# Channel attention with a feed-forward layer: keys issued from one queue, and a first chunk of one row

## The chip, the cores and the metric

The kernel runs on one core of a Trainium2 chip. The metric is the device time of one execution in microseconds (us), the median of several executions. The kernel before takes 1074.12 us (three runs, 1074.07 to 1074.76).

The engines are called PE (matrix multiplication), ACT (activations and copies), DVE and POOL (elementwise work), and SP, which here only issues DMA transfers. PEld is the weight load that goes ahead of each matmul. "ACTq" and "SPq" rows are the issuing of transfers by these engines.

## What is computed

```
q, k, v: (2, 6016, 256) float32;  w_in: (256, 2048);  w_out: (2048, 256)
qn = q / (norm of q over axis 1 + 1e-6);  kn likewise
s  = kn^T @ qn / tau                 # (2, 256, 256), one matrix per batch
a  = softmax of s over the last axis
x  = v @ a                           # (2, 6016, 256), seen as 12032 tokens
h  = x @ w_in;  out = (h * sigmoid(h)) @ w_out
```

## The kernel before, in words

The program has two parts. The **scoring part** (to about 84 us of the span) reads all queries and keys once, adds up the 256 x 256 scores and the sums of squares for the norms. The **token part** (the rest) folds the softmax of each batch into w_in and sends the tokens through both layers in 12 steps of 8 pairs of matrix products. In the token part the order of each engine's work is fixed, and PE's matmuls follow each other.

In the scoring part a batch has 47 "rows": a row is 128 partitions x 256 channels of the queries and the same of the keys, 128 KB each. Rows go in chunks. `HEADS` (L55) gives the rows of a batch's first chunks and every other chunk has 3 rows, so batch 0 is cut into 2, 3, 3, ... (16 chunks) and batch 1 likewise; chunks are numbered 0 to 31 and called c0, c1, ... here. A chunk's queries are one transfer and its keys another, into one of 9 slots of a ring (the slots carry the names qk, wp_raw and home in the trace: chunk 5 and 6 go to wp_raw, 7 and 8 to home, then 9 to 13 to qk, and so on). From c9 on a load waits until the chunk nine before has been scored and squared.

All transfers of the scoring part are issued by SP (L287 queries, L289 keys), but for the keys of c0, c1 and c2, which ACT issues before its first work (L770 and L771, `KEYS_BY_ACT = 3`). Behind some chunks SP also issues parts of w_in, tau and the first tokens (`W_IN_BEHIND`, `TAU_BEHIND`, `TOKENS_BEHIND`, all chunk numbers).

For each chunk in order, ACT squares queries and keys into PSUM (L630), and DVE adds the squares to a running sum (L846); the two take turns over two PSUM areas. PE scores a chunk in one of two ways. A plain chunk takes two float32 matmuls of 256 columns per row (L434, each shown as two records). A **split** chunk (the keys of `LATE`: 5, 8, 11, 14, 17, 20, 21, 23, 27) is rounded by ACT (L676), its remainder is taken by POOL (L354), and PE scores it from the parts (L449 to L456). `LATE[g]` says after how many further chunks PE comes back to it: c5 is scored behind c7, c14 behind c15.

Before any data is there, PE runs `WARM = 7` float32 matmuls of a matrix of ones by itself (L585; 14 records), whose result nothing reads.

Of the kernel before, what the change touches and what calls it, by code (L numbers as in the profile page):

```python
# [11 lines left out]
P = 128  # L12
BANK = 512
# [3 lines left out]
TOK = 512  # L17
NARROW = 448

KEYS_BY_ACT = 3  # L20
WARM = 7


LATE = {5: 2, 8: 2, 11: 2, 14: 1, 17: 3, 20: 2, 21: 5, 23: 5, 27: 4}
SPLIT = tuple(LATE)

W_IN_BEHIND = (17, 24, 26, 28)
TAU_BEHIND = 11
TOKENS_BEHIND = 22
SETS = 2  # L30


# [8 lines left out]
def channel_attention_ffn(nc, q, k, v_t, tau, w_in, w_out, out_t):  # L41
# [6 lines left out]
    B, N, C = q.shape  # L48
    F = w_in.shape[1]
    CK = C // P  # L50
    FK = F // P
    PAIRS = FK // 2
    R = N // P

    HEADS = ((2,), (2,))  # L55
    CHUNKS = []
    for b in range(B):
        row = 0
        for rows in HEADS[b] + (ROWS,) * ((R - sum(HEADS[b])) // ROWS):
            CHUNKS.append((b, row, rows))  # L60
            row += rows
        assert row == R
    ENDS = [sum(b <= last for b, _, _ in CHUNKS) for last in range(B)]
    SECOND = ENDS[0]

    ORDER = sorted(range(len(CHUNKS)), key=lambda g: (g + LATE[g], 1) if g in SPLIT else (g, 0))
    PLACE = [ORDER.index(g) for g in range(len(CHUNKS))]
    assert all(CHUNKS[g][2] == ROWS and CHUNKS[g][0] == CHUNKS[g + LATE[g]][0] for g in SPLIT)
    assert [g for g in ORDER if g in SPLIT] == list(SPLIT)
    WIDE = N // (2 * TOK)  # L70
    STEPS = WIDE + 1
    ALL = B * STEPS
    FOLDS = CK * (F // BANK)
    PARTS = 4
    assert B == 2 and N % P == 0 and N == 2 * (TOK * WIDE + NARROW) and NARROW % 2 == 0
    assert C == 2 * P and PAIRS == 8 and FOLDS == 8 and F == PARTS * BANK and STEPS == 6 and ENDS == [16, 32] and TOK <= BANK

    with ExitStack() as ctx:
        def sb(name, shape, dt=F32, stack=ctx):
            return stack.enter_context(nc.sbuf_tensor(name, shape, dt))  # L80

        def sem(name):
            return ctx.enter_context(nc.semaphore(name))
# [40 lines left out]
        with ExitStack() as early:  # L124
            qk = [sb(f"qk{s}", [P, 2, ROWS, C], stack=early) for s in range(RING - 4)]
# [60 lines left out]
        slot_loaded = [sem(f"slot_loaded{s}") for s in range(RING)]  # L186
# [63 lines left out]
        def rows_of(x, g):  # L250

            b, row, rows = CHUNKS[g]
            return x[b, row * P:(row + rows) * P, :].rearrange("(p r) c -> p r c", r=rows)
# [6 lines left out]
        def w_in_part(w, n):  # L260
            return w[:, :, n * BANK:(n + 1) * BANK]

        def tokens_of(step):

            return 2 * TOK * (step % STEPS), TOK if step % STEPS < WIDE else NARROW
# [10 lines left out]
        @block.sync  # L276
        def _(sp):
            def load_chunk(g):
                rows = CHUNKS[g][2]
                s = g % RING  # L280
                if g >= RING:
                    if g - RING in SPLIT:
                        sp.wait_ge(rows_split, SPLIT.index(g - RING) + 1)
                    else:
                        sp.wait_ge(chunk_scored, PLACE[g - RING] + 1)
                    sp.wait_ge(chunk_squared, 2 * (g - RING + 1))
                sp.dma_start(qk[s][:, 0, 0:rows, :], rows_of(q, g)).then_inc(slot_loaded[s], 16)  # L287
                if g >= KEYS_BY_ACT:
                    sp.dma_start(qk[s][:, 1, 0:rows, :], rows_of(k, g)).then_inc(slot_loaded[s], 16)  # L289

            def load_v(step):

                first, n = tokens_of(step)
                for i, (c, t) in enumerate(((0, 1), (0, 0), (1, 0), (1, 1))):
                    sp.dma_start(v_raw[:, i, 0:n], v_t[step // STEPS, c * P:(c + 1) * P,
                                                       first + t * n:first + (t + 1) * n]).then_inc(v_loaded, 16)

            sp.sem_inc(out_stored, 32)
            w_out_parts = w_out.rearrange("(n f p) c -> n p f c", p=P, n=PARTS)
            w_in_parts = w_in.rearrange("(c p) (n f) -> n p c f", p=P, f=BANK)  # L300
            for g in range(len(CHUNKS)):
                load_chunk(g)
                if g in W_IN_BEHIND:
                    n = W_IN_BEHIND.index(g)
                    sp.dma_start(w_in_part(w_in_raw, n), w_in_parts[n]).then_inc(w_in_loaded[n], 16)
                if g == TAU_BEHIND:
                    sp.dma_start(tau_col[:], bass.AP(tau.tensor, 0, [[0, P], [1, 1]])).then_inc(tau_loaded, 16)
                if g == TOKENS_BEHIND:
                    load_v(0)
            for n in range(PARTS):  # L310
                sp.dma_start(wo_raw[:, n * FK // PARTS:(n + 1) * FK // PARTS, :], w_out_parts[n]).then_inc(
                    wo_loaded[n], 16)
            sp.wait_ge(v_split, 3)
            load_v(1)

            def out_half(step, t):
                first, n = tokens_of(step)
                first += step // STEPS * N + t * n
                return out_t.rearrange("(c p) n -> p c n", p=P)[:, :, first:first + n]

            for step in range(ALL - 1):

                n = tokens_of(step)[1]
                for late, t in enumerate((1, 0)):
                    sp.wait_ge(out_copied, 2 * step + late + 3)
                    sp.dma_start(out_half(step, t), out_sb[:, t, :, 0:n]).then_inc(out_stored, 16)
                if step < ALL - 2:

                    sp.wait_ge(out_stored, 32 * step + 64)
                    load_v(step + 2)  # L330
            for late, t in enumerate((1, 0)):
                last = out_half(ALL - 1, t)
                sp.wait_ge(last_copied_dve, late + 1)
                sp.dma_start(last[:, 0, :], out_sb[:, t, 0, 0:NARROW]).then_inc(out_stored, 16)
                if late == 0:
                    sp.wait_ge(last_copied_act, 1)
                    sp.dma_start(last[:, 1, :], out_sb[:, t, 1, 0:NARROW]).then_inc(out_stored, 16)

            sp.wait_ge(out_stored, 32 * ALL + 64)
# [87 lines left out]
        def _(pe):  # L427
# [155 lines left out]
            pe.wait_ge(consts_made, 1)  # L583
            for n in range(WARM):
                nc.tensor.matmul(ps_turn[:, 0:P], ones[:], ones[:], start=True, stop=True)  # L585
# [37 lines left out]
        def _(act):  # L623
# [143 lines left out]

            act.sem_inc(silu_11, 1)
            act.sem_inc(out_copied, 2)
            for g in range(KEYS_BY_ACT):  # L770
                act.dma_start(qk[g][:, 1, 0:CHUNKS[g][2], :], rows_of(k, g)).then_inc(slot_loaded[g], 16)  # L771
            for g in range(len(CHUNKS)):
                square_chunk(g)
                if g in SPLIT:
# [286 lines left out]
```

## Time and profile before

| what | value |
|---|---|
| median of three runs | 1074.12 us |
| the profiled execution, its own time | 1073.79 us |
| its span in the profile | 1072.0 us |
| PE busy | 1067.4 us of the span |
| DVE, ACT, POOL busy | 729.7, 633.8, 61.9 us |
| moved by DMA | 54.08 MB, 361, 398 and 358 GB/s in the first three of 40 slices |

The span begins with the first instruction that the profiler records and ends with the last; the execution's own time has 1.79 us more around it. POOL's work lies in the scoring part alone. A row of a timeline gives the start, the time from the first start to the last end of the merged instructions, the engine, the line, the operation with its tiles, and in brackets how long the engine had been idle before and what ended the wait. Ends of matmuls are modelled, so neighbouring PE rows overlap a little.

### The profile page before, as it was taken

What the parts mean: (1) busy time and instruction counts of PE and PEld (TensorE: products, weight loads), DVE (VectorE), ACT (ScalarE), POOL (GpSimd) and SP (SyncE); (2) the same over time, 40 slices, a digit from 0 to 9 for tenths busy, and PEclk for the clock granted to TensorE, in tenths of its full rate; (3) what the DMA queues carried; (4) which work ended last, traced back from release to release, by engine and by line L of the source; (5) the groups of instructions that cost most, each with busy time, mean ns of one, the idle gap of its engine ahead of it and who ended that gap; (6) DMA issues with size and microseconds to landing.
All of it is one profiled execution on the core that took longest, in us unless ns stands there. A gap on an engine that the chain in (4) does not pass through costs nothing.

```text
span 1072.0 us, 13049 instructions
## 1 busy us (share of the span) xinstructions
PE 1067.4 (100%) x4850; PEld 902.8 (84%) x4850; DVE 729.7 (68%) x939; ACT 633.8 (59%) x787; POOL 61.9 (6%) x33
## 2 busy tenths in 40 slices
PE   9999999999999999999999999999999999999998
PEld 8988888888888888888999888888888888888998
DVE  6889787567566566566788776667567566566665
ACT  7998665555555555555666655555555555555554
POOL 3692000000000000000000000000000000000000
PEclk9999999999999999999999999999999999999999
DMA  9991000200200200200200200200200200200100
GB/s 361 398 358 40 1 1 1 79 1 1 79 1 0 78 0 0 73 0 0 80 1 0 74 1 1 79 1 1 79 1 1 78 0 0 73 0 0 40 1 35
DMA packets 26077, 54.08 MB, mean 50 GB/s; under 512 B 2480, under 2 KB 6576, under 8 KB 26032
## 3 DMA queue, kind: packets, MB, share of 16 engines
q1 hardware_dynamic: 25456, 52.21, 13.4%
q10 hardware_dynamic: 576, 1.28, 0.3%
q8 instruction: 27, 0.44, 0.2%
q14 instruction: 18, 0.15, 0.0%
HBM read 41.16 MB, written 12.32 MB: 50 GB/s over the span
## 4 chain that ended last, share of the span: by engine, by line
PE 99%; DMA 1%; ACT 0%; ACTq 0%; issue 0%
PE ps_o L529 16%; PE ps_o L530 16%; PE ps_o L531 16%; PE ps_h L495 14%; PE ps_h L496 14%; PE ps_h L494 14%; PE ps_o L434 5%; PE ps_o L449 1%; PE ps_o L456 1%; DMA qk<-k_dram 1%; PE ps_h L486 0%; PE ps_h L488 0%; PE ps_h L487 0%; PE ps_o L488 0%; PE ps_o L487 0%; PE ps_o L486 0%
## 5 line engine op out<-in xcount | busy, mean ns | idle before, releaser
L496 PE MATMUL ps_h<-b_hi,a_lo_rest 128*128 128x512 f32 (+1 forms) x504 | 194.1, 385 | 0.0
L495 PE MATMUL ps_h<-b_lo,a_hi_rest 128*128 128x512 f32 (+1 forms) x504 | 194.1, 385 | 0.0
L494 PE MATMUL ps_h<-b_hi,a_hi_rest 128*128 128x512 f32 (+1 forms) x504 | 194.0, 385 | 0.0
L978 DVE TENSOR_TENSOR h_b<-ps_h,u 128x512 f32<-128x512 f32 x96 | 66.4, 692 | 161.5 <-PE ps_h L496 161.4
L956 DVE TENSOR_TENSOR u<-ps_h,u 128x512 f32<-128x512 f32 x96 | 66.4, 692 | 142.9 <-PE ps_h L496 91.7
L750 ACT ACTIVATE h_a<-ps_h 128x512 f32<-128x512 f32 x96 | 57.4, 598 | 161.9 <-PE ps_h L496 161.8
L530 PE MATMUL ps_o<-g_lo_a,wo_hi 128*128 128x512 f32 (+1 forms) x384 | 147.9, 385 | 0.0
L529 PE MATMUL ps_o<-g_hi_b,wo_hi 128*128 128x512 f32 (+1 forms) x384 | 147.9, 385 | 0.0
L531 PE MATMUL ps_o<-g_hi_b,wo_lo 128*128 128x512 f32 (+1 forms) x384 | 147.9, 385 | 0.0
L529 PE MATMUL ps_o<-g_hi_a,wo_hi 128*128 128x512 f32 (+1 forms) x384 | 147.9, 385 | 0.0
L530 PE MATMUL ps_o<-g_lo_b,wo_hi 128*128 128x512 f32 (+1 forms) x384 | 147.8, 385 | 0.0
L531 PE MATMUL ps_o<-g_hi_a,wo_lo 128*128 128x512 f32 (+1 forms) x384 | 147.8, 385 | 0.0
L760 ACT ACTIVATE h_b<-h_b 128x1024 f32<-128x1024 f32 x96 | 102.0, 1063 | 42.6 <-DVE h_b L980 42.6
L728 ACT ACTIVATE u<-ps_h 128x512 f32<-128x512 f32 x96 | 57.3, 597 | 115.8 <-PE ps_h L496 115.7
L982 DVE TENSOR_TENSOR g_lo_a<-h_a,g_hi_a 128x1024 fp32r<-128x1024 f32 x96 | 116.8, 1217 | 1.6 <-ACT g_hi_a L754 1.6
L949 DVE TENSOR_TENSOR g_lo_b<-h_b,g_hi_b 128x1024 fp32r<-128x1024 f32 x95 | 115.4, 1215 | 0.0
L747 ACT ACTIVATE h_a<-h_a 128x512 f32<-128x512 f32 x96 | 60.8, 633 | 91.5 <-DVE h_a L963 91.3
L494 PEld LDWEIGHTS ps_h<-b_hi,a_hi_rest 128*128 128x128 f32 x504 | 94.6, 188 | 17.7
L496 PEld LDWEIGHTS ps_h<-b_hi,a_lo_rest 128*128 128x128 f32 x504 | 94.6, 188 | 17.6
L495 PEld LDWEIGHTS ps_h<-b_lo,a_hi_rest 128*128 128x128 f32 x504 | 94.6, 188 | 17.6
L754 ACT ACTIVATE g_hi_a<-h_a 128x1024 fp32r<-128x1024 f32 x96 | 101.9, 1062 | 4.6
L705 ACT ACTIVATE g_hi_b<-h_b 128x1024 fp32r<-128x1024 f32 x95 | 100.1, 1054 | 0.0
(140 smaller groups left out, 1601.3 us busy)
## 6 DMA issues: line engine op xcount, KB each, us to landing
v_raw<-v_t_dram SPq DMA_DIRECT2D x40, 256.0 KB, 3.6
out_t_dram<-v_raw SPq DMA_DIRECT2D x20, 512.0 KB, 3.2
qk<-q_dram SPq DMA_DIRECT2D x19, 384.0 KB, 10.6
qk<-k_dram SPq DMA_DIRECT2D x17, 384.0 KB, 12.2
wp_raw<-q_dram SPq DMA_DIRECT2D x6, 384.0 KB, 10.3
wp_raw<-k_dram SPq DMA_DIRECT2D x6, 384.0 KB, 10.9
w_in_raw<-w_in_dram SPq DMA_DIRECT2D x4, 512.0 KB, 11.9
wo_raw<-w_out_dram SPq DMA_DIRECT2D x4, 512.0 KB, 12.3
```

What stands on the lines that cost most here:

```text
L494: nc.tensor.matmul(ps_h[:, bank, 0:n], w_hi, x_hi, start=start, stop=False, skip_group_check=True)
L495: nc.tensor.matmul(ps_h[:, bank, 0:n], w_hi, x_lo, start=False, stop=False, skip_group_check=True)
L496: return nc.tensor.matmul(ps_h[:, bank, 0:n], w_lo, x_hi, start=False, stop=stop, skip_group_check=True)
L529: nc.tensor.matmul(out, wo_hi[:, block_, d], g_hi[:, i, 0:tok], start=start, stop=False)
L530: nc.tensor.matmul(out, wo_hi[:, block_, d], g_lo[:, i, 0:tok], start=False, stop=False)
L531: return nc.tensor.matmul(out, wo_lo[:, block_, d], g_hi[:, i, 0:tok], start=False, stop=stop)
L705: nc.scalar.activation(g_hi_b[:], h_b[:], ACT.Copy).then_inc(hi_b, 1)
L754: nc.scalar.activation(g_hi_a[:], h_a[:], ACT.Copy).then_inc(hi_a, 1)
L760: nc.scalar.activation(h_b[:], h_b[:], ACT.Silu).then_inc(silu_b, 1)
L949: nc.vector.tensor_tensor(g_lo_b[:], h_b[:], g_hi_b[:].bitcast(F32), ALU.subtract).then_inc(lo_b, 1)
L956: nc.vector.tensor_tensor(u[:], ps_h[:, BANK_P6, :], u[:], ALU.add).then_inc(u_made, 1)
L982: nc.vector.tensor_tensor(g_lo_a[:], h_a[:], g_hi_a[:].bitcast(F32), ALU.subtract).then_inc(lo_a, 1)
```

## The change

Three things, with the tables of chunk numbers moved along. All keys are issued by SP, each behind its chunk's queries. Batch 0 opens with chunks of 1, 2 and 2 rows in place of 2 and 3, so that it has 17 chunks, and every later chunk keeps its rows and gets a number one higher (c2 before is n3 now; chunks of the changed kernel are called n0, n1, ... here). PE runs five matmuls of ones ahead, not seven.

```diff
-KEYS_BY_ACT = 3
-WARM = 7
-LATE = {5: 2, 8: 2, 11: 2, 14: 1, 17: 3, 20: 2, 21: 5, 23: 5, 27: 4}
+WARM = 5
+LATE = {6: 2, 9: 2, 12: 2, 15: 1, 18: 3, 21: 2, 22: 5, 24: 5, 28: 4}
...
-W_IN_BEHIND = (17, 24, 26, 28)
-TAU_BEHIND = 11
-TOKENS_BEHIND = 22
+W_IN_BEHIND = (18, 25, 27, 29)
+TAU_BEHIND = 12
+TOKENS_BEHIND = 23
...
-    HEADS = ((2,), (2,))
+    HEADS = ((1, 2, 2), (2,))
...
                 sp.dma_start(qk[s][:, 0, 0:rows, :], rows_of(q, g)).then_inc(slot_loaded[s], 16)
-                if g >= KEYS_BY_ACT:
-                    sp.dma_start(qk[s][:, 1, 0:rows, :], rows_of(k, g)).then_inc(slot_loaded[s], 16)
+                sp.dma_start(qk[s][:, 1, 0:rows, :], rows_of(k, g)).then_inc(slot_loaded[s], 16)
...
-            for g in range(KEYS_BY_ACT):
-                act.dma_start(qk[g][:, 1, 0:CHUNKS[g][2], :], rows_of(k, g)).then_inc(slot_loaded[g], 16)
```

On SP, at the start of the program, the order before is this (128x512 is two rows, 128x768 three):

```order
L287 DMA qk<-q_dram 128x512
L287 DMA qk<-q_dram 128x768 x3
L289 DMA qk<-k_dram 128x768
L287 DMA qk<-q_dram 128x768
L289 DMA qk<-k_dram 128x768
L287 DMA wp_raw<-q_dram 128x768
```

And the same place on SP in the changed program:

```order
L286 DMA qk<-q_dram 128x256
L287 DMA qk<-k_dram 128x256
L286 DMA qk<-q_dram 128x512
L287 DMA qk<-k_dram 128x512
L286 DMA qk<-q_dram 128x512
L287 DMA qk<-k_dram 128x512
L286 DMA qk<-q_dram 128x768
L287 DMA qk<-k_dram 128x768
```

SP now issues queries and keys in turn from the first chunk on, and has issued six transfers with five rows where it had issued four with eleven rows of queries.

On ACT, at the start of the program, before:

```order
L771 DMA qk<-k_dram 128x512
L771 DMA qk<-k_dram 128x768 x2
L630 ACT_TABLE_LOAD
L630 ACTIVATE ps_h<-qk 128x512 x2
L630 ACTIVATE ps_h<-qk 128x768 x8
```

And the same place on ACT in the changed program:

```order
L628 ACT_TABLE_LOAD
L628 ACTIVATE ps_h<-qk 128x256 x2
L628 ACTIVATE ps_h<-qk 128x512 x4
L628 ACTIVATE ps_h<-qk 128x768 x4
```

The three issues ahead of the table load are gone, and the squares come in three small chunks and then in chunks of three rows.

## Rows read from the trace of the kernel before

**Rows 1.** The page: busy time of each engine over the span.
```profile
PE 1067.4 (100%) x4850; PEld 902.8 (84%) x4850; DVE 729.7 (68%) x939; ACT 633.8 (59%) x787; POOL 61.9 (6%) x33
```

**Rows 2.** Waits of PE: whom it waited for, us in total, times, longest.
```profile
PE ps_o L585 <- POOL ones L343: 1.1, 1, 1.1
PE ps_o L434 <- DMA qk<-k_dram: 0.4, 2, 0.2
```

**Rows 3.** Timeline of PE, the opening.
```profile
1.07 3.33 PE L585 MATMUL ps_o<-ones 128*128 128x128 f32 x14 [1.07 <-POOL ones L343]
4.57 1.99 PE L434 MATMUL ps_o<-qk 128*128 128x256 f32 x8 [0.17 <-DMA qk<-k_dram]
6.78 10.63 PE L434 MATMUL ps_o<-qk 128*128 128x256 f32 x48 [0.21 <-DMA qk<-k_dram]
17.24 2.75 PE L434 MATMUL ps_o<-wp_raw 128*128 128x256 f32 x12
```

**Rows 4.** Timeline of SP's and ACT's issuing, the opening.
```profile
0.81 1.81 SPq L287 DMA_DIRECT2D qk<-q_dram  x4
0.89 1.35 ACTq L771 DMA_DIRECT2D qk<-k_dram  x3
2.66 0.74 SPq L289 DMA_DIRECT2D qk<-k_dram  x1
4.89 0.43 SPq L289 DMA_DIRECT2D wp_raw<-k_dram  x1
5.84 0.43 SPq L289 DMA_DIRECT2D wp_raw<-k_dram  x1
```

**Rows 5.** DMA issues by short windows: size, us to landing; c0, c1, c2 from ACT.
```profile
qk<-k_dram ACTq DMA_DIRECT2D x1, 256.0 KB, 3.6
...
qk<-k_dram ACTq DMA_DIRECT2D x1, 384.0 KB, 5.4
...
qk<-k_dram ACTq DMA_DIRECT2D x1, 384.0 KB, 7.0
```

**Rows 6.** The same for SP's keys of c3, c5 and c6.
```profile
qk<-k_dram SPq DMA_DIRECT2D x1, 384.0 KB, 7.8
...
wp_raw<-k_dram SPq DMA_DIRECT2D x1, 384.0 KB, 9.4
...
wp_raw<-k_dram SPq DMA_DIRECT2D x1, 384.0 KB, 10.5
```

**Rows 7.** Tile v_raw at 87 to 95 us: four 256 KB loads on idle queues.
```profile
L295 SPq DMA_DIRECT2D v_raw<-v_t_dram x4: 340/432/432, 88.6 to 89.9; - x4
...
DMA to landing us min/median/max: 2.6/3.3/4.5
```

**Rows 8.** Timeline of ACT: table load, squares of c0, c2 and c5.
```profile
2.27 1.28 ACT L630 ACT_TABLE_LOAD   x1 [2.27 <-issue]
4.55 1.12 ACT L630 ACTIVATE ps_h<-qk 128x512 f32<-128x512 f32 x2 [1.00 <-DMA qk<-k_dram]
...
8.78 1.55 ACT L630 ACTIVATE ps_h<-qk 128x768 f32<-128x768 f32 x2 [0.48 <-DMA qk<-k_dram]
...
14.48 0.81 ACT L630 ACTIVATE ps_h<-wp_raw 128x768 f32<-128x768 f32 x1 [0.28 <-DVE square_sum L846]
```

**Rows 9.** Timeline of POOL: the remainders of c14, and of c20 with c21.
```profile
37.70 3.48 POOL L354 TENSOR_TENSOR qk_parts<-wp_raw,qk_parts 128x1536 fp32r<-128x1536 f32 x1 [3.22 <-ACT qk_parts L676]
...
52.24 6.95 POOL L354 TENSOR_TENSOR qk_parts<-qk,qk_parts 128x1536 fp32r<-128x1536 f32 x2 [1.60 <-ACT qk_parts L676]
```

**Rows 10.** Timeline of PE's weight loads: the first of c14, the first of c20.
```profile
41.62 0.19 PEld L452 LDWEIGHTS ps_o<-qk_parts 128*128 128x128 f32 x1
...
56.27 0.19 PEld L449 LDWEIGHTS ps_o<-qk_parts 128*128 128x128 f32 x1
```

**Rows 11.** Weight loads by tile: count, ns min/median/max, first and last start.
```profile
L585 PEld LDWEIGHTS ps_o<-ones x14: 289/333/338, 1.0 to 3.8; 128*128 128x128 f32 x14
...
L434 PEld LDWEIGHTS ps_o<-qk x33: 186/190/190, 4.6 to 11.8; 128*128 128x128 f32 x33
```

**Rows 12.** Mean granted clock by windows (after the PE, PEld, DVE, ACT, POOL columns).
```profile
3.00:4.00 1.00, 1.00 (x7) 1.00 (x6) 0.00 (x0) 0.55 (x1) 1.00 (x1) 1.00 0.98 381
4.00:5.00 1.00, 0.83 (x4) 0.51 (x4) 0.00 (x0) 0.45 (x1) 0.25 (x1) 1.00 1.04 413
```

More of the change, by code:

```diff
@@ L75, in channel_attention_ffn @@
     assert B == 2 and N % P == 0 and N == 2 * (TOK * WIDE + NARROW) and NARROW % 2 == 0
-    assert C == 2 * P and PAIRS == 8 and FOLDS == 8 and F == PARTS * BANK and STEPS == 6 and ENDS == [16, 32] and TOK <= BANK
+    assert C == 2 * P and PAIRS == 8 and FOLDS == 8 and F == PARTS * BANK and STEPS == 6 and ENDS == [17, 33] and TOK <= BANK
     with ExitStack() as ctx:
```

## The prediction

> **What bounds the kernel now.** The page comes first: PE is busy for 1067.4 of 1072.0 us [rows 1], so only 4.6 us of the span are PE's idle time, and no change of order can win more than that without removing matmuls. The list of PE's waits comes next: it holds three waits only, one of 1.1 us for the ones to be written and 0.4 us, in two pieces, for keys [rows 2]. The timeline says where they lie. PE multiplies ones until 4.40, scores c0 from 4.57 and c1 from 6.78, and from there never waits again: c1 to c4, four chunks with 12 rows, take 6.78 to 17.24, which is 0.872 us a row and 2.615 a chunk [rows 3]. So the end of the kernel is the time at which PE's unbroken stream starts, plus its work. This change leaves the work as it is (the same 94 rows, the same parts) and can only move the start. The rest of the argument is whether what feeds PE (transfers, then ACT's rounding, then POOL's remainders) can follow if PE comes earlier.
>
> **When the data lands now.** A landing is the issue time plus the time to landing. ACT issues its three keys from 0.89, 0.45 us apart [rows 4], and they land at 4.49 (c0), 6.74 (c1) and 8.79 (c2) [rows 5]; PE at 4.57 and 6.78 and ACT's squares at 8.78 start just there [rows 3, 8]. Keys from SP: c3 at 2.66 + 7.8 = 10.46, c5 at 4.89 + 9.4 = 14.29, c6 at 5.84 + 10.5 = 16.34 [rows 4, 6]. From c3 to c6 nine rows arrive in 5.88 us: 0.653 us a row. That is a stream that is full all the time, and the change moves the same bytes through it. Carried back from c3 (11 rows landed), the line gives 8.50 for 8 rows, 6.54 for 5, 5.24 for 3 and 3.93 for one. What really landed was 0.3 and 0.2 us behind this line for c2 and c1, since queries of later chunks went beside their keys.
>
> **The change, part by part.**
>
> *Keys from SP, in order.* The keys of n0, n1, n2 and n3 are SP's 2nd, 4th, 6th and 8th issues. Four issues took 1.81 us [rows 4], 0.45 each, so n1's keys go out at 0.81 + 3 x 0.45 = 2.17 where those of c1 went at 1.34. For their landing no row exists; the bounds are 2.17 + 2.6 = 4.77, by the quickest of four loads of 256 KB on idle queues [rows 7], and 6.74, where c1's keys landed now. I take 5.24, by the line of the full stream, since it also meets c0 (4.58 for two rows against 4.49 measured). In the same way n0 is complete at 3.93, n2 at 6.54 and n3 at 8.50. Against the move speaks only the issuing. The Trainium skill (DMA: Bandwidth & Descriptors, "Issuing engines are not separate DMA queues") says that issuing on several engines saves just the sequencer's time and that all transfers share the same 16 DMA engines; by that rule nothing is lost, and the sum stays. SP's own queue gets five more issues ahead of n7's, about 2.3 us; they are covered by the backlog, as c6's keys waited 10.5 us [rows 6] and leave about 7.9 now to land at 16.34. Without that backlog all starts behind would be up to 2.3 us later.
>
> *Chunks of 1, 2 and 2 rows.* PE starts n0 at 3.93. Its row costs 0.87 at the full clock and 1.74 at half; if the clock rises at about 4.3 it ends at 5.0, before n1 is there. n1 runs from 5.24 to 6.98, n2 (landed 6.54) to 8.73, n3 (landed 8.50) starts at 8.73. Before, the same rows (c2) start at 6.78 + 2.615 = 9.40. **Gain at the front: 0.67 us.** It is n1's landing that sets this, not n0's. The added chunk costs PE nothing and ACT about 0.7 us of squares (1.12 for two rows, 1.55 for three [rows 8]), DVE about as much, between 3.9 and 5.2, where both wait for n1. The table load begins near 0.9 in place of 2.27 and ends before n0 lands either way: nothing. n9's new wait is on n0, done long before. The shifted tables name the same data as before: nothing.
>
> *Five pairs of ones.* Each record took 0.214 us, so ten end near 3.55 in place of 4.40, before n0 lands. Nothing is won but that they are out of n0's way; with seven pairs n1 would still wait for 5.24. What it may cost is in the rivals.
>
> *Does the rest follow?* c6 starts at 17.24 and landed at 16.34: 0.90 us of room, enough for 0.67. The split chunks are tighter. POOL's remainder of c14 ends at 37.70 + 3.48 = 41.18 and PE's first weight load of it is at 41.62: 0.44. For c20 it is 52.24 + 3.48 = 55.72 and 56.27: 0.55 [rows 9, 10]. POOL waits for ACT there, and ACT squares c5 at 14.48, when its keys had landed at 14.29: ACT can come 0.19 earlier and no more, as the transfers do not come sooner. So PE can gain 0.44 + 0.19 = 0.63 at c14. With a little slower start of a single queue taken off, I put **the net at 0.55 us**: what is late next is POOL's remainder of c14, on which PE waits for the first time. Behind 84 us everything hangs on PE's own stream and shifts with it.
>
> **Sum.** Against the profiled execution: 1073.79 - 0.55 = 1073.24. The median of the runs stands 0.33 above that execution, so **1073.6 us**. A measurement of this kernel can tell about 0.2%, 2.15 us, from no change; the forecast is inside that.
>
> **The rivals.**
>
> *The clock rises late (slower).* The granted clock reads 1.00 from the start [rows 12], but the weight loads tell otherwise: 333 ns for the ones, 190 from c0's first on, with one of 289 last among the ones [rows 11]. So PE ran at 1.2 GHz until about 4 us and at 2.4 from 4.57, after more than 3 us of unbroken matmuls. Now it would be busy from 1.07 to 3.55 and have holes at 3.55 to 3.93 and before n1. With the rise at time T, n0 takes 3.93 to 5.67, and n1 and n2 (3.49 us of work) end at 6.33 + T/2; against 9.40 that is a loss from T = 6.15 on. A rise 3.5 us late, at 8.0, ends them at 10.33: 0.9 lost, 1075.0. Only from T = 10.5 would the loss pass 2.15. For it: fewer ones and the holes. Against it: the holes are short, and real matmuls go on. The Trainium skill (TensorE: Matmul & The Clock Gate, "Part 1") says that the default state is throttled and activity releases it, which would make this the danger of the change. Chance 0.10, and 0.03 of them beyond 10.5.
>
> *The single queue starts slower.* SP's first two issues carry 128 KB each in 0.45 us, 0.29 MB/us, under the 0.40 at which the stream then runs. If the whole line is 0.4 us later, n1 starts at 5.64, the front gains 0.27, and c14 leaves 0.44 - 0.21 = 0.23: 1073.9 to 1074.1. At the upper bound of n1's landing (6.74, the line 1.5 late) 0.8 is lost. The Trainium skill's rule (DMA: Bandwidth & Descriptors, "Rules for kernel authors") to use 1 MiB or more per transfer for bandwidth speaks for this rival; the trace has nothing under 256 KB here. Chance 0.17.
>
> *More than the forecast.* Small transfers on otherwise idle queues land nearer to 4.8 for n1, and POOL and ACT give more room than their modelled ends show. Then the front gains up to 0.90, where c6's landing stops it: 1073.1. Chance 0.13.
>
> *The change does not do what it says.* n0 may land no sooner than c0 did, 4.49, if a landing is mostly latency. Then n0 ends at 5.36, n1 starts 0.1 later, and the net is 0.5 still: no time of its own.
>
> **How the numbers follow.** Forecast 0.57, more 0.13, slow queue 0.17, late clock 0.10, and 0.03 for what I do not see. All but the far end of the late clock lie within 2.15 us, and the largest gain the rows allow is under 1 us: faster 0.02, same 0.94, slower 0.04. The range holds forecast, slow queue, more, and most of the late clock with the runs' own spread of 0.3: 1072.8 to 1074.9.
>
> **What would show it.** PE's row of n0 near 3.9, of n1 near 5.2, of n3's rows near 8.7; the landings of SP's keys on the line 3.93, 5.24, 6.54, 8.50. A first wait of PE for POOL at c14 (n15 now), of a tenth or two, and ACT's squares of n6 at 14.3. Weight loads of 190 ns from the second half of n0 on. The prediction is wrong if n1's keys land after 6, if weight loads of 333 ns go on past n1, or if PE waits more than half a microsecond for POOL or ACT.

## The result, and the profile after

The changed kernel takes **1075.97 us** (median of 22 runs, 1075.11 to 1076.51) where the kernel before takes 1074.13 (22 runs, 1073.57 to 1074.76): 1.84 us slower, a ratio of 1.0017 with the interval 1.001 to 1.0023. The forecast was 1073.6, with a range to 1074.9. The time lies outside it and went the other way. The loss is inside the 0.2% up to which the forecast spoke of "same", but the interval leaves out a ratio of 1, so it is a loss and not noise. The profiled execution took 1076.3 us with a span of 1074.5, 2.5 us more span than before.

PE's list of waits in the changed kernel (us in total, times, longest), where [rows 2] stood before:

```profile
PE ps_o L432 <- DMA qk<-k_dram: 1.2, 2, 0.9
PE ps_o L583 <- POOL ones L341: 1.1, 1, 1.1
PE ps_o L472 <- ACT scores L645: 0.6, 1, 0.6
PE ps_o L461 <- DVE square_sum L848: 0.3, 1, 0.3
```

Two waits are new, both far behind the chunks that were changed: for ACT's exponentials and for DVE's sum of squares, in the softmax of batch 1. The opening of PE, in answer to [rows 3]:

```profile
1.07 2.47 PE L583 MATMUL ps_o<-ones 128*128 128x128 f32 x10 [1.07 <-POOL ones L341]
3.36 1.91 PE L432 MATMUL ps_o<-qk 128*128 128x256 f32 x4
5.66 3.72 PE L432 MATMUL ps_o<-qk 128*128 128x256 f32 x16 [0.39 <-DMA qk<-k_dram]
10.23 5.45 PE L432 MATMUL ps_o<-qk 128*128 128x256 f32 x24 [0.85 <-DMA qk<-k_dram]
15.51 2.75 PE L432 MATMUL ps_o<-wp_raw 128*128 128x256 f32 x12
```

n0 starts at 3.36, even sooner than forecast, and n1 at 5.66. But n3, the first chunk of three rows, starts at 10.23: 1.5 us later than forecast and about 0.8 later than the same rows (c2) before, which start at 9.40 by the forecast's working and at 9.47 by their first record. The cause is to be read from the landings. These are the keys of n0 to n4 from SP's queue, each asked for in its own short window (KB, us to landing), as [rows 5, 6]:

```profile
qk<-k_dram SPq DMA_DIRECT2D x1, 128.0 KB, 2.1
...
qk<-k_dram SPq DMA_DIRECT2D x1, 256.0 KB, 3.4
...
qk<-k_dram SPq DMA_DIRECT2D x1, 256.0 KB, 4.1
...
qk<-k_dram SPq DMA_DIRECT2D x1, 384.0 KB, 6.1
...
qk<-k_dram SPq DMA_DIRECT2D x1, 384.0 KB, 7.1
```

Issued at 1.25, 2.18, 3.13, 4.08 and 5.03, they land at 3.35, 5.58, 7.23, 10.18 and 12.13. The forecast line had 3.93, 5.24, 6.54, 8.50 and 10.46. So one row came earlier, and from three rows on each landing is later, up to 1.7 us for 8 and 11 rows. The windows of the opening (last column GB/s, the one before it the share of the DMA engines that is busy) show a thin stream where it had 381, 413, 406, 415 and 403 GB/s from 3 to 8 us before:

```profile
3.00:4.00 1.00, 1.00 (x5) 0.81 (x5) 0.17 (x1) 0.67 (x2) 1.00 (x1) 1.00 0.72 178
4.00:5.00 1.00, 1.00 (x4) 0.62 (x2) 0.59 (x2) 0.03 (x1) 0.25 (x1) 1.00 1.05 399
5.00:6.00 1.00, 0.61 (x4) 0.32 (x3) 0.00 (x0) 0.37 (x1) 0.00 (x0) 1.00 0.94 292
6.00:7.00 1.00, 1.00 (x6) 0.90 (x5) 0.73 (x2) 0.75 (x2) 0.00 (x0) 1.00 1.08 373
7.00:8.00 1.00, 1.00 (x7) 0.87 (x6) 0.70 (x2) 0.78 (x2) 0.00 (x0) 1.00 0.94 341
```

Only a part of this is idle time of the DMA engines: their busy shares add up to 4.73 of these 5 us in place of 5.10 before, 7% less, while the bytes are 22% fewer (1.58 MB in place of 2.02). The rest is packets that took longer. From 9 us on the stream moves as fast as before, but what it missed stays missed. Added up, the windows to 8 us have moved 1.87 MB in place of 2.27. These 0.40 MB are 1.0 us of the full stream, so the thin stream makes about 1.0 of the 1.67 us by which the keys of 11 rows are late. For the rest, 3.56 MB had moved by that landing where it was 3.28 MB before: bytes of later chunks went ahead of it. ACT squares n6 at 16.12 where c5 had 14.48, and POOL takes every remainder 1.56 us later. At n15, the c14 of [rows 9, 10], the room of 0.44 us is gone (timelines of POOL and of the weight loads):

```profile
39.26 3.48 POOL L352 TENSOR_TENSOR qk_parts<-wp_raw,qk_parts 128x1536 fp32r<-128x1536 f32 x1 [3.25 <-ACT qk_parts L674]
...
42.80 0.19 PEld L450 LDWEIGHTS ps_o<-qk_parts 128*128 128x128 f32 x1 [0.27 <-POOL qk_parts L352]
```

PE waits 0.27 us there and is 1.06 us late behind it (n17 at 45.05 where c16 had 43.99). At the last split chunk it is 1.10 late (82.22 against 81.12). The other 1.4 us of the 2.5 arise between 82 and 97 us. This is DVE, then POOL, before (the last squares are added until 81.2, L851 and L852 add up the three rows, L878 begins the softmax sums of batch 0; POOL's L396, L366 and L401 take remainders that PE needs later):

```profile
81.20 2.05 DVE L851 TENSOR_TENSOR square_sum<-square_sum 128x512 f32<-128x512 f32 x1
83.28 0.69 DVE L852 TENSOR_TENSOR square_sum<-square_sum 128x512 f32<-128x512 f32 x1
83.89 2.37 DVE L878 TENSOR_SCALAR row_sum<-row_sum 128x2 f32<-128x2 f32 x1
```

```profile
80.29 2.41 POOL L396 TENSOR_TENSOR b_lo<-t_raw,b_hi 128x1024 fp32r<-128x1024 f32 x1
83.63 2.60 POOL L366 TENSOR_TENSOR w_in_lo<-w_in_raw,w_in_hi 128x1024 fp32r<-128x1024 f32 x1 [0.94 <-ACT w_in_hi L686]
86.19 2.37 POOL L401 TENSOR_TENSOR b_lo<-v_raw,b_hi 128x1024 fp32r<-128x1024 f32 x1
```

And the same in the changed kernel (L847 and L848 are the additions, L874 the softmax sums):

```profile
82.26 2.54 DVE L847 TENSOR_TENSOR square_sum<-square_sum 128x512 f32<-128x512 f32 x1
84.84 2.81 DVE L848 TENSOR_TENSOR square_sum<-square_sum 128x512 f32<-128x512 f32 x1
87.57 2.33 DVE L874 TENSOR_SCALAR row_sum<-row_sum 128x2 f32<-128x2 f32 x1
```

```profile
81.87 2.38 POOL L394 TENSOR_TENSOR b_lo<-t_raw,b_hi 128x1024 fp32r<-128x1024 f32 x1
84.69 2.40 POOL L364 TENSOR_TENSOR w_in_lo<-w_in_raw,w_in_hi 128x1024 fp32r<-128x1024 f32 x1 [0.44 <-ACT w_in_hi L684]
87.06 2.81 POOL L399 TENSOR_TENSOR b_lo<-v_raw,b_hi 128x1024 fp32r<-128x1024 f32 x1
```

Compare the durations. One addition over 128x512 takes 0.69 us by itself. When one of POOL's instructions is under way as it starts, it ends 0.55 us after POOL's does (83.25 and 82.70, 87.65 and 87.09), and so takes 2.05 to 2.81 us here. A sum over 128x2 takes 2.3 us in the same company, ends 0.03 us after POOL's instruction, and takes 0.16 alone, as an experiment below shows. POOL's instruction is the longer one when it comes second: 2.60 us for L366 at 83.63 and 2.81 for L399 at 87.06, where the others of this size take about 2.4. So the two engines take turns. Before, the second addition started at 83.28, in the gap that POOL left between 82.70 and 83.63; it missed POOL's next instruction by 0.35 us. In the changed kernel POOL leaves only 0.44 us (84.25 to 84.69), the first addition ends behind the gap, and the second waits for a whole instruction of POOL, the third for one more. DVE's scaling of the scores begins at 90.72 in place of 87.71, the exponentials at 95.19 in place of 92.18, and PE, which had folds to do meanwhile, runs out of them at 95.8. The Trainium skill (SBUF — State Buffer, "Who interferes with whom") states this as a rule: DVE and GpSimd (POOL here) share one pair of SBUF ports as an exclusive lock, a DVE instruction with two SBUF inputs contends for it with a GpSimd instruction that reads SBUF, and so does DVE in a two-port mode, where whoever issues first blocks the other for the whole instruction. The trace agrees, with 0.69 against 2.81 us.

### The profile page after: what moved, and what is told of

Its sections match the earlier page's. It is cut to its first block, busy times and chain, and to the rows that moved or that the text cites. A ratio compares the mean times of both kernels' runs of the same rounds, so it can differ in the third digit from the quotient of the medians.

```text
span 1074.5 us, 13051 instructions
## 1 busy us (share of the span) xinstructions
PE 1068.1 (99%) x4846; PEld 902.2 (84%) x4846; DVE 732.1 (68%) x941; ACT 633.7 (59%) x789; POOL 62.1 (6%) x33
## 4 chain that ended last, share of the span: by engine, by line
PE 91%; ACT 4%; DVE 2%; issue 1%; DMA 1%; SPq 1%; ACTq 0%
PE ps_o L527 16%; PE ps_o L528 16%; PE ps_o L529 16%; PE ps_h L493 14%; PE ps_h L494 14%; PE ps_h L492 14%; ACT ps_h L628 3%; DVE square_sum L842 1%; DMA wp_raw<-k_dram 1%; ACT qk_parts L674 0%; PE ps_o L486 0%; PE ps_o L484 0%; PE ps_o L485 0%; SPq L286 0%; DVE square_sum L848 0%
## 6 DMA issues: line engine op xcount, KB each, us to landing
wp_raw<-q_dram SPq DMA_DIRECT2D x7, 384.0 KB, 10.4
w_in_raw<-w_in_dram SPq DMA_DIRECT2D x4, 512.0 KB, 11.5
```

## The experiments

Medians are of 11 runs each; the kernel before had 1074.03, 1074.11 and 1073.96 in the three sets, of 33 runs each. The brackets give the ratio to it and the ratio's interval, which is about 0.001 wide on either side, 1 us, so that differences are read together with the traces. Three theories stood at first. *One queue* and *small chunks* say that the transfers come late, by the one or the other part of the change; *clock* says that fewer ones cost it.

**Keys from SP alone.** Chunks and ones as before.

```diff
-KEYS_BY_ACT = 3
+KEYS_BY_ACT = 0
```

> The kernel before, with all keys issued by SP behind their queries, chunks of 2 and 3 rows and seven pairs of ones as before. Theory 'one queue' (the transfers of the first microseconds run dry because one engine issues them all): 1.0 to 2.0 us slower than before, c3's keys land after 11.2 us where they landed at 10.5. Theory 'small chunks' (an issue takes 0.45 us whatever it carries, so 128 and 256 KB transfers leave holes): within 0.4 us of before. Theory 'clock': within 0.4 us of before, no weight load of 333 ns after 5 us.

Measured: 1074.84 (1.0005, 0.9996 to 1.0015). PE's opening, and three windows of the transfers:

```profile
4.44 2.55 PE L434 MATMUL ps_o<-qk 128*128 128x256 f32 x8
8.48 10.63 PE L434 MATMUL ps_o<-qk 128*128 128x256 f32 x48 [1.49 <-DMA qk<-k_dram]
```

```profile
4.00:5.00 1.00, 1.00 0.94 266
5.00:6.00 1.00, 1.00 1.09 277
6.00:7.00 1.00, 1.00 0.78 277
```

(The windows have only the granted clock, the share and the GB/s.) c1 starts at 8.48 where it started at 6.78, and the stream is thin there with transfers of 256 and 384 KB too. So this edit alone makes the first landings late: c3's keys land at 12.36 us, past the 11.2 that this theory named. The median is 0.81 us above before, less than the profile's 1.7 us (the profiled execution took 1075.53) and less than the theory wanted, and the interval still holds a ratio of 1. The edit changes two things at once, the queue of three transfers and the order in which queries and keys enter (each chunk's keys now go ahead of the next chunk's queries); no run separates them. Each issue carries 256 KB or more in 0.47 us here, above the rate of the stream, so the pace of issuing is not what makes the stream thin.

**Small chunks alone.** The heads of the change, keys of the first three chunks by ACT, seven pairs of ones.

```diff
-    HEADS = ((2,), (2,))
+    HEADS = ((1, 2, 2), (2,))
```

> The kernel before, with batch 0 opening with chunks of 1, 2 and 2 rows, keys of the first three chunks still issued by ACT, seven pairs of ones. Theory 'one queue': no slower than before, perhaps 0.5 us faster. Theory 'small chunks': 1.0 to 2.0 us slower, the keys of the fourth chunk (8 rows in) land after 9.5 us. Theory 'clock': within 0.4 us of before.

Measured: 1074.81 (1.0009, 1.0 to 1.0019). PE's row of n2:

```profile
8.52 7.17 PE L434 MATMUL ps_o<-qk 128*128 128x256 f32 x32 [0.24 <-DMA qk<-k_dram]
```

n2 starts at 8.52 and n3 two rows later, against 9.40 for the same rows before; the keys of 11 rows land at 11.5 in place of 10.46. The keys of 8 rows land at 9.55, at the edge of what the theory of small chunks named. So this part makes the landings late too; the median is 0.78 us above before, less than the theory wanted, with an interval that begins at 1. Neither theory is right alone, and neither part gains anything.

**Five pairs of ones alone.**

```diff
-WARM = 7
+WARM = 5
```

> The kernel before with five pairs of ones in place of seven, nothing else. Theories 'one queue' and 'small chunks': within 0.2 us of before. Theory 'clock' (fewer ones let the clock rise later, and this is what the change costs): 1 to 2 us slower, weight loads of 333 ns in the first chunk.

Measured: 1075.69 (1.0015, 1.0006 to 1.0024), none of its 11 runs below 1074.98. The weight loads up to 10 us, and PE's row:

```profile
L434 PEld LDWEIGHTS ps_o<-qk x13: 288/332/338, 4.7 to 9.6; 128*128 128x128 f32 x13
...
4.72 15.33 PE L434 MATMUL ps_o<-qk 128*128 128x256 f32 x56 [1.17 <-DMA qk<-k_dram]
```

The ones end at 3.55, PE stands for 1.17 us, and then its weight loads take 332 ns until 10.8: it ran at 1.2 GHz for six more microseconds, and c6 came 2.65 us late (19.89 against 17.24). This is the forecast's rival of the late clock, but in another kernel.

**The change with seven pairs.**

```diff
-WARM = 5
+WARM = 7
```

> The changed kernel with seven pairs of ones as before. Theories 'one queue' and 'small chunks': as slow as the changed kernel, about 1076.0 us, within 0.3 us. Theory 'clock': back to 1074.5 us or less.

Measured: 1076.10 (1.0018, 1.0009 to 1.0027). The clock theory falls for the change itself: with two pairs more the time is the same. In the changed kernel PE goes from the ones straight to n0, and its weight loads take 190 ns from 5.65 on. In it ACT and POOL are later than PE (1.64 and 1.56 us against 0.8).

A second set asked which lateness costs the time. *Late feeders*: ACT, DVE and POOL are late, and PE waits for them. *PE alone*: only PE's start and clock count.

**ACT late, all else as before.** One copy whose result nothing uses:

```diff
                 act.wait_ge(slot_loaded[g % RING], 32 * (g // RING + 1))
+                if g == 2:
+                    nc.scalar.activation(qk_parts[1][:, 0], qk[g][:, :, :, :], ACT.Copy)
```

> The kernel before, with one more copy of 1,536 columns on ACT (about 1.47 us) ahead of the squares of c2, whose result nothing uses; transfers, chunks and ones as before. Theory 'late feeders' (in the changed kernel ACT, DVE and POOL run 1.56 us late because the first chunks land late, and PE, though itself less late, waits for them at c14 and in the softmax of batch 1): 1.0 to 1.8 us slower than before; PE waits for DVE's sum of squares and for ACT's exponentials after 86 us, as in the changed kernel. Theory 'PE alone' (only PE's own start and its clock count, the feeders have room): within 0.3 us of before, no such waits.

Measured: 1076.14 (1.0019, 1.001 to 1.0028): all of the change's loss, and slightly more than expected, with the landings of before (10.5 us for 11 rows). All 11 runs lie within 0.5 us. In the profile c6 on PE is 0.56 us late; that is not the copy but PE's clock, whose slow weight loads went on to 6.8 us here and to 4.1 in the profile of before. DVE, then POOL, in the tail:

```profile
84.79 2.80 DVE L854 TENSOR_TENSOR square_sum<-square_sum 128x512 f32<-128x512 f32 x1
```

```profile
84.63 2.41 POOL L366 TENSOR_TENSOR w_in_lo<-w_in_raw,w_in_hi 128x1024 fp32r<-128x1024 f32 x1 [0.42 <-ACT w_in_hi L688]
```

The same rows as in the changed kernel, within 0.06 us.

**A shorter tail, before and changed.** The squares of one late chunk are cut to 8 columns:

```diff
+                    width = 8 if g == SECOND + 12 else C
+                    tall = 1 if g == SECOND + 12 else rows
...
-                    nc.scalar.activation(ps_squares[i][:, 0:rows, :], qk[g % RING][:, i, 0:rows, :],
+                    nc.scalar.activation(ps_squares[i][:, 0:tall, 0:width], qk[g % RING][:, i, 0:tall, 0:width],
```

and DVE's addition likewise. The norms of batch 1 leave these rows out.

> The kernel before, with the squares of c28 and their addition cut to 8 columns of one row each (its norms of batch 1 leave these rows out), which frees about 1.5 us of ACT and as much of DVE ahead of the softmax of batch 1. It is the control of the next run. Theory 'late feeders': within 0.3 us of before, or up to 0.4 faster, since PE did not wait there. Theory 'PE alone': the same.

Measured: 1074.18. Nothing, as expected.

> The changed kernel with seven pairs of ones and with the squares of n29 and their addition cut to 8 columns of one row each (its norms of batch 1 leave these rows out). Theory 'late feeders': the waits of PE for DVE's sum and ACT's exponentials go, and with them 0.7 to 1.3 us against the same kernel uncut (1076.1): 1074.8 to 1075.4. Theory 'PE alone': as slow as uncut, within 0.3 us.

Measured: 1074.16 (1.0003, 0.9994 to 1.0012): 1.94 us less than uncut, more than expected, and level with the kernel before. The waits for DVE and ACT are gone from PE's list. So the tail is where the change loses its time. The theory of PE alone falls. In this profile n3 starts at 9.85, in those of the other kernels with the changed opening at 9.97 to 10.75: the front's lateness differs from one execution to the next.

**The change without the move of the keys.** Keys of the first three chunks by ACT, five pairs of ones, small chunks.

> The changed kernel with the keys of its first three chunks issued by ACT again; chunks of 1, 2 and 2 rows and five pairs of ones stay. Theory 'late feeders' (keys from one queue and small chunks each make the first transfers later, and the clock matters little as long as the feeders are later): 1074.8 to 1075.6. Theory 'PE alone': the clock after five pairs decides, as in the kernel before with five pairs: 1075.7 or more.

Measured: 1075.19 (1.0012, 1.0003 to 1.0021), within what late feeders gave. Its profiled execution took only 1074.29 and its runs spread from 1074.29 to 1076.17. In that profile the keys of 11 rows land at 11.2 and DVE's second addition takes 0.69 us, so it does not show what the slower runs lost.

A third set asked what in the tail costs 1.4 us when the feeders are 1.56 late: *plain lateness*, or the *missed slot* on DVE.

**POOL waits for DVE's sum.**

```diff
             split_t12()
+            pool.wait_ge(rows_added[1], 1)
             split_w_in(3)
```

In the changed kernel:

> The changed kernel, where POOL waits for the end of DVE's sum over the rows of batch 1 before it takes the remainder of the last part of w_in; nothing else. Theory 'missed slot' (DVE's second addition has to begin in the gap before POOL's remainder at 84.7 us, the change closes that gap, and DVE then stands behind two of POOL's instructions for 2 us each): the second addition takes 0.7 us again, PE's waits for DVE's sum and ACT's exponentials go, 1.2 to 1.9 us faster than the changed kernel: 1074.1 to 1074.8. Theory 'plain lateness' (the whole chain is as late as its feeders, whoever blocks whom): within 0.4 us of the changed kernel, or slower, since POOL comes later still.

Measured: 1074.92 (1.0007, 0.9998 to 1.0016): 1.05 us won by making POOL wait, against 1075.97 without. That is less than the 1.2 to 1.9 expected. DVE, then POOL:

```profile
84.62 0.69 DVE L849 TENSOR_TENSOR square_sum<-square_sum 128x512 f32<-128x512 f32 x1
85.23 0.16 DVE L875 TENSOR_SCALAR row_sum<-row_sum 128x2 f32<-128x2 f32 x1
```

```profile
85.39 2.39 POOL L364 TENSOR_TENSOR w_in_lo<-w_in_raw,w_in_hi 128x1024 fp32r<-128x1024 f32 x1 [1.35 <-DVE square_sum L849]
```

POOL starts 0.7 us later than in the changed kernel (84.69), DVE's two instructions take 0.85 us together where they took 5.1, and PE waits for neither DVE nor ACT any more. Plain lateness falls.

> The same with seven pairs of ones. Theory 'missed slot': 1074.0 to 1074.7, and the difference from the run with five pairs is what the clock costs inside this change: up to 0.5 us. Theory 'plain lateness': about 1076.0.

Measured: 1075.00 (1.0009, 1.0 to 1.0018), 0.08 from the run with five pairs: inside this change the ones cost nothing that can be told. What it expected of the time, 1074.0 to 1074.7, was too low as for five pairs.

> The kernel before with the extra copy on ACT (1076.14 without this wait), where POOL waits for DVE's sum in the same place. Theory 'missed slot': 1074.3 to 1074.8, since PE itself was only 0.2 us late in that kernel up to c14. Theory 'plain lateness': 1075.8 or more.

Measured: 1074.71 (1.0007, 0.9998 to 1.0016): 1.43 us won back in a kernel whose transfers, chunks and ones are those of before, within what the missed slot gave. The slot is the tail's cost there too.

**Eight pairs of ones in the kernel before.**

> The kernel before with eight pairs of ones. If seven pairs leave the rise of the clock to luck in some runs, the eighth makes it sooner or surer and costs nothing, since c1 is waited for anyway: 1073.8 to 1074.1, with no run above 1074.8. If the clock is always up by c0: 1074.1 to 1074.3, as the ones now end at 4.8 us and c0 starts there.

Measured: 1074.15 (1.0002, 0.9993 to 1.0011), runs from 1073.61 to 1075.20. The number fits the second case, but its ground does not: the clock was not up by c0, slow weight loads (337 ns) went on to 6.3 us. No gain: no kernel of this study beats the one before.

## Why the prediction was wrong, by its own steps

*What bounds the kernel, and that work stays as it is:* right in the main. PE's busy time is 1068.1 us, 0.7 more than before, and the other 1.8 of the 2.5 us are idle time of PE.

*"That is a stream that is full all the time", carried back to one row:* **the first step that failed.** The line came from landings between 10 and 16 us of a kernel whose first transfers were 256 KB and more on two queues. With one queue, or with smaller first transfers, the stream is not full between 3 and 8 us. n1 came 0.34 us late by the line, n2 0.7, n3 1.7. The front was to gain 0.67 and lost about 0.8. The upper bound for n1's landing held (6.74, and 5.58 was measured), but it was put on the wrong chunk: n3 decides, not n1. The rival of the slow single queue had this mechanism, with 0.8 us lost as its end, and a chance of 0.17, too small. Two kernels show that each part does it alone, so it is not just the queue. The rule of the Trainium skill that the forecast leaned on (DMA: Bandwidth & Descriptors, "Issuing engines are not separate DMA queues"), that issuing from several engines saves only the sequencer's time, does not account for the opening of this kernel: with keys from SP alone the stream moved 266 to 277 GB/s from 4 to 7 us in place of 406 to 415, though its issues were ahead of it, and c1's start went from 6.78 to 8.48 in the profile. The measurement decides, though it does not say whether the queue or the order of the transfers did it.

*"Behind 84 us everything hangs on PE's own stream and shifts with it":* **the step that made the error large.** The tail had room of 0.35 us on an engine that the forecast had not looked at. POOL runs almost without a gap from 52 us to 84 and keeps its lateness; ACT, which has waits for PE on the way (for a buffer at 54.09 before, 0.49 us), ends with about PE's. What closes the gap is the difference: POOL's L396 starts 1.58 us late and ACT's copy ahead of L366 1.06 (before, then changed), so about 0.5 of the gap's 0.94 goes, more than 0.35.

```profile
82.51 1.04 ACT L686 ACTIVATE w_in_hi<-w_in_raw 128x1024 fp32r<-128x1024 f32 x1
...
83.57 1.04 ACT L684 ACTIVATE w_in_hi<-w_in_raw 128x1024 fp32r<-128x1024 f32 x1
```

With keys from SP alone both are late by 1.7, the second addition takes 0.69 us, and the tail costs nothing. The forecast would have met this edge even if its front had come true: PE, and with it ACT, 0.6 earlier and POOL only 0.19 closes the gap by about 0.4. That is worked out and was not run.

*The waits at c14:* the right place, but by luck. PE's first wait for POOL is there, 0.27 us, where a tenth or two was forecast. It was to arise because PE came 0.67 us earlier and POOL only 0.19; it arose because POOL came 1.56 late and PE about 0.8, which uses up the 0.44 of room.

*The new issues ahead of n7:* a small slip. With c6's keys landing 10.5 us after 5.84, 2.3 us more of issuing leave 8.2 of backlog, not 7.9; nothing hangs on it.

*Five pairs of ones cost nothing here:* right for this change, by two pairs of runs (1076.10 and 1075.97, 1075.00 and 1074.92). The danger of the rival is real in the kernel before, 1.66 us. What the profiles show to differ ahead of the clock's rise is the hole before the first chunk: 1.17 us there, none here. That this hole decides is argued; no run varied it alone. The rival read one thing wrong: the weight load of 289 ns among the ones is the first (at 1.04 us) and not the last, which takes 333 at 3.78, so the ones show no sign of the rise.

*Squares of the added chunk, the shifted tables, n9's wait:* nothing in the profile speaks against their zero.

The 2.5 us of the profiled span are then about 0.8 at n3, 0.3 up to 82 us with the wait at n15 in it, and 1.4 in the tail. The runs confirm the tail: undoing it gives back 1.05, 1.10 and 1.43 us with POOL's wait, and 1.94 with the cut squares. What stays over the kernel before is 0.96 and 1.04 us in the first two, about the front's share, but 0.05 in the cut one, although its landings are late too (11.7 us for 11 rows). How much of the front's lateness reaches the median is therefore **open**. Open too is why the first transfers come late: the windows show a thin stream, the pace of issuing is ruled out for whole chunks by the keys-alone run, and no run took the slow transfers apart. The packet records show where the time goes, and not why. From 3 to 8 us, 13 packets of 2 to 3 KB took over 0.4 us in the changed kernel, the longest 1.09, where the median is 0.08; in the kernel before none did there.

## What to carry to other kernels

A stage that PE fills without a gap is not thereby free of other edges: before a start is moved, look behind the stage for the narrowest gap between two engines that block each other, not only for waits of PE. A landing time may be carried on along a full stream, but not back into its first microseconds, where here the queue or order of the transfers, and their size, each moved it by a microsecond or more. Where a DVE instruction takes four times its usual duration, lay POOL's rows beside it; one wait that lets the short instruction go first gave back 1.05 to 1.43 us here.

## What the runs showed of the hardware that was not expected

- Two additions of DVE and a sum over 128x2 took 2.3 to 2.8 us beside POOL's instructions and take 0.69 and 0.16 without them. The cost is a step: with 0.35 us of room nothing is lost, and 0.15 us too late is 2 us on DVE.
- In the opening a core's transfers ran at 178 to 373 GB/s in four of five microseconds where they had run at 381 to 415. The landing of 11 rows was at 10.4 to 10.6 us in the six profiles with unchanged transfers, and at 11.2 to 12.6 in the eight with keys from SP alone, small chunks, or both.
- Single slow packets go with it. In the six profiles with unchanged transfers the packets over 0.4 us (5 to 21 of them) all start before 3 us; from 3 to 8 us none takes over 0.39. In the eight others 5 to 26 start between 3 and 8 us, and the longest take 0.7 to 1.6 us.
- With five pairs of ones in the kernel before, PE stood for 1.17 us after 2.5 us of ones, and its clock stayed at the lower level to 10.8 us, though PE then worked almost all the time. In the thirteen other profiles the slow weight loads end between 4.0 and 7.3 us, and not at one time for one opening: at 4.1 in the kernel before, at 6.3 to 6.8 in three kernels with its transfers and seven or eight pairs, where c6 starts 0.4 to 0.6 us later. The granted clock in the windows reads 1.00 throughout; the duration of weight loads (332 or 190 ns) tells the level.
